# An attention and two-MoE kernel: scores before transposes, score moves joined two and two, routing steps spread over three heads, last output scaled by ScalarE

## What is computed

```python
# attention: q, k, v are (2, 8, 1152, 64); queries are averaged in pairs -> 576
q_pool = q.reshape(B, H, S // 2, 2, D).mean(axis=3)
scores = np.matmul(q_pool, k.transpose(0, 1, 3, 2)) / np.sqrt(D)
attn = softmax(scores)                       # over the 1152 keys
x = (attn @ v) -> (1152 tokens, 512)
# first MoE: the best of 8 experts for each token, at most 288 tokens each
expert_idx = np.argmax(x @ w_gate, axis=1); gate_w = softmax value of it
out[i] = gate_w[i] * (relu(x[i] @ w1[e]) @ w2[e])
# second MoE: all 8 experts for all tokens, weights balanced in 8 rounds
out += P[:, e:e + 1] * (relu(x @ w1[e]) @ w2[e])
```

## Time and profile before

| | |
|---|---|
| median of 3 runs | 1281.7 us (1281.13 to 1282.16) |
| the profiled execution's own time | 1281.55 us |
| its span | 1279.8 us |
| busy: TensorE matmul / weight load | 1247.5 us (97%) / 1167.1 us (91%) |
| busy: VectorE, ScalarE, GpSimd | 713.7 us (56%), 550.2 us (43%), 644.3 us (50%) |
| attention | 0 to about 277 us of the span |
| last head's routing, scatter and reload | about 273 to 292 us |
| the two MoE stages | from about 292 us to the end |
| granted TensorE clock, mean | 0.993 |

### The profile page before, as it was taken

The page is one execution under the profiler, slowest core; times in us unless marked ns, Lnnn a source line. Parts: engine busy times, 40 slices in busy tenths (PEclk is TensorE's granted clock), DMA queues, the critical chain, the costliest instruction groups (busy, mean ns, idle before and its releaser), DMA issues.

```text
span 1279.8 us, 23007 instructions
## 1 busy us (share of the span) xinstructions
PE 1247.5 (97%) x8056; PEld 1167.1 (91%) x8056; DVE 713.7 (56%) x1759; ACT 550.2 (43%) x1220; POOL 644.3 (50%) x529
## 2 busy tenths in 40 slices
PE   7999999968999999999999999999999999999998
PEld 6999999968999999988989989988998998998996
DVE  8999999972222222687654534534544543543552
ACT  6787777765665543323223322312412421422320
POOL 6655557519888764545335334344443532533512
PEclk9999999998999999999999999999999999999999
DMA  4364433237665652011101101001011010110101
GB/s 123 114 191 143 143 100 127 85 98 253 167 172 190 185 171 67 34 34 66 34 33 67 33 33 66 33 33 66 33 53 45 33 66 33 33 66 33 33 0 68
DMA packets 72452, 107.26 MB, mean 84 GB/s; under 512 B 7206, under 2 KB 38758, under 8 KB 72384
## 3 DMA queue, kind: packets, MB, share of 16 engines
q1 hardware_dynamic: 67792, 97.29, 23.3%
q10 hardware_dynamic: 2816, 4.72, 2.1%
q0 software_dynamic: 1776, 4.37, 0.9%
HBM read 94.92 MB, written 11.81 MB: 83 GB/s over the span
## 4 chain that ended last, share of the span: by engine, by line
PE 93%; DVE 3%; ACT 2%; issue 1%; DMA 1%; POOLq 0%; DVEq 0%; ACTq 0%
PE psum L1664 30%; PE psum L1711 26%; PE psum L1594 8%; PE psum L1577 7%; PE psum L1428 6%; PE psum L1438 6%; PE psum L1453 5%; PE psum L1653 2%; PE psum L1471 1%; ACT wsplit L696 1%; PE psum L1566 1%; DVE raw L980 1%; DVE acts L989 1%; ACT acts L696 0%; DVE small L980 0%
## 5 line engine op out<-in xcount | busy, mean ns | idle before, releaser
L1664 PE MATMUL psum<-wsplit,acts 128*128 128x512 f32 x1728 | 396.6, 390 | 0.0
L1664 PEld LDWEIGHTS psum<-wsplit,acts 128*128 128x128 f32 x1728 | 323.0, 188 | 66.1
L1711 PE MATMUL psum<-acts,wsplit 128*128 128x288 f32 x1800 | 260.9, 295 | 0.0
L1711 PEld LDWEIGHTS psum<-acts,wsplit 128*128 128x128 f32 x1800 | 247.2, 188 | 1.1
L653 POOL TENSOR_TENSOR wsplit<-raw,wsplit 128x512 fp32r<-128x512 f32 x64 | 85.9, 1365 | 297.8 <-ACT wsplit L696 297.8
L1392 DVE SCALAR_TENSOR_TENSOR x<-psum,eqr,x 128x512 f32<-128x512 f32 x126 | 94.6, 751 | 234.2 <-PE psum L1664 234.2
L643 POOL TENSOR_TENSOR wsplit<-raw,wsplit 128x512 fp32r<-128x512 f32 x109 | 140.1, 1323 | 139.6 <-ACT wsplit L696 139.6
L934 ACT ACTIVATE acts<-psum 128x288 fp32r<-128x288 f32 x240 | 92.2, 410 | 193.3 <-DVE psum L1358 118.3
L696 ACT ACTIVATE acts<-psum 128x384 fp32r<-128x384 f32 (+2 forms) x304 | 120.1, 448 | 115.8 <-PE psum L1594 56.0
L696 ACT ACTIVATE wsplit<-raw 128x512 fp32r<-128x512 f32 x301 | 169.6, 623 | 0.1
L941 ACT ACTIVATE raw<-psum 128x288 f32<-128x288 f32 x60 | 24.4, 407 | 299.8 <-PE psum L1711 299.8
(11 more groups left out here) (168 smaller groups left out, 1476.0 us busy)
## 6 DMA issues: line engine op xcount, KB each, us to landing
raw<-in_moe_w_dram SPq DMA_DIRECT2D x32, 1024.0 KB, 5.4
raw<-in_moe_w_dram SPq DMA_DIRECT2D x64, 512.0 KB, 4.2
raw<-in_k_dram SPq DMA_DIRECT2D x15, 576.0 KB, 3.7
raw<-in_q_dram SPq DMA_DIRECT2D x15, 576.0 KB, 3.9
raw<-in_v_dram SPq DMA_DIRECT2D x16, 288.0 KB, 4.5
slots_in<-zero SPq DMA_DIRECT2D x3, 1536.0 KB, 8.7
x<-slots_in ACTq DMA_DIRECT2D x7, 576.0 KB, 7.0
out_dram<-zero SPq DMA_DIRECT2D x3, 768.0 KB, 6.5
```

The costliest lines, as they stand in the source:

```text
L1664: last = mm(psum[:, bank, :], hs[a][:, l, tile * P:(tile + 1) * P], w2f[z][:, l, :], start=(l == 0 and (a, z) == (0, 0)), stop=(l == LF - ...
L1711: last = mm(psum[:, bank, 0:QN], w1f[a][:, x, cc, i * P:(i + 1) * P], src(z, cc), start=(not adds and cc == 0 and (a, z) == (0, 0)), stop= ...
```

## The change

The PSUM banks are laid out anew: `RING` becomes (0, 1, 2, 3), so that two chunks of a tile lie in neighbouring banks; the transposes take banks 4 to 6, the values bank 7. move_scores takes two chunks in one instruction and the third in another: for t below 4 chunks 0 and 1 together, then 2; for t = 4 chunk 0, then 1 and 2 together. TensorE issues scores(t + 2) before turn_probs(t); ScalarE issues exps(t + 1) before p_hi(t); VectorE issues both moves of tile t + 2 before the three p_lo(t). The transposes of the last tile take 64 rows and a 64 x 64 identity. In the routing of group 0, `one_hot` goes from head 9 t = 2 to head 10 t = 0, `slot_limit` from head 9 t = 4 to head 10 t = 1, `scatter_index` from head 10 t = 4 to head 11 t = 0. In the last head's routing `gate_input` goes ahead of `mark_expert`, `scale_output` goes from VectorE to ScalarE (one activation for each tile, after scale_logits), and `prefix(1)` goes behind the last value product. No DMA is added or removed.

```diff
...
         rs, rsr, cs, csr, gm = keep[:, 0:NT], drop[:, 0:NT], held, base[:, 0:E], pos[:, 0:4]
         g11 = den[0:1, 0:1]
         psum = ctx.enter_context(nc.psum_tensor("psum", [P, 8, 512], F32))
-        BPT, TBANKS, BPV = 3, 3, 6
-        RING = (0, 1, 2, 7)
+        BPT, TBANKS, BPV = 4, 3, 7
+        RING = (0, 1, 2, 3)
+        MOVES = ((0, 2), (2, 1))
+        MOVES_LAST = ((0, 1), (1, 2))
...
+                    if not (last and t == QT - 1):
+                        exps(*ahead(g, v, t, 1))
                     for c in range(NC):
                         p_hi(g, v, t, c)
                         if c == 0 and t == QT - 1:
                             if first:
                                 act.wait_ge(consts, 21)
                             row_sums(g)
-                    if not (last and t == QT - 1):
-                        exps(*ahead(g, v, t, 1))
...
+            def scale_output(group, bank):
+                act.wait_ge(den_done, G)
+                act.wait_ge(lgh_done, G + group - 1)
+                for n in range(*GROUPS[group]):
+                    t = n - QT
+                    last = nc.scalar.activation(x[:, t, (G - 1) * DH:G * DH], psum[:, bank, t * FD:t * FD + DH],
+                                                ACT.Copy, scale=den[:, t:t + 1])
+                last.then_inc(x_done, 1)
...
             exps(0, 0, 0)
             over_heads(head)
             evac_ot(G - 1, 0)
+            scale_output(1, BTURN)
             exp_gate(1)
             evac_ot(G - 1, 1)
             scale_rows(1)
+            scale_output(2, BTURN2)
             exp_gate(2)
             scale_rows(2)
...
-            def move_scores(g, v, t, c):
+            def move_scores(g, v, t, i):
                 b = buf(v, t)
+                c, n = (MOVES if t < QT - 1 else MOVES_LAST)[i]
+                bank = s_bank(t, c)
+                assert s_bank(t, c + n - 1) == bank + n - 1
                 if c == 0 and not (is_first(g) and t < NP):
                     dve.wait_ge(pt_ready, SCH * g + NC * (t - NP + 1))
                 if c:
                     dve.wait_ge(s_moved, SCH * g + NC * t + c)
-                dve.wait_ge(s_ready, SCH * g + NC * t + c + 1)
-                nc.vector.tensor_scalar(prob[b][:, c * CH:(c + 1) * CH], psum[:, s_bank(t, c), 0:CH],
-                                        QSCALE, low[:, b, c - 1:c] if c else None, ALU.mult, ALU.min,
-                                        accum_out=low[:, b, c:c + 1]).then_inc(s_moved, 1)
+                dve.wait_ge(s_ready, SCH * g + NC * t + c + n)
+                nc.vector.tensor_scalar(prob[b][:, c * CH:(c + n) * CH].rearrange("p (a k) -> p a k", a=n),
+                                        psum[:, bank:bank + n, 0:CH],
+                                        QSCALE, low[:, b, 0:1] if c else None, ALU.mult, ALU.min,
+                                        accum_out=low[:, b, NC - 1:NC] if c else low[:, b, 0:1]).then_inc(s_moved, n)
 
...
             def head(g, v):
                 first, last = is_first(g), is_last(g)
                 for t in range(QT):
+                    for i in (0, 1):
+                        if not (last and t >= QT - 2):
+                            move_scores(*ahead(g, v, t, 2), i)
+                    if g == CHOOSE0 and t == 1:
+                        mark_expert(0)
+                        gate_input(0)
+                    if g == PLACE0 and t == 0:
+                        one_hot(0)
+                    if g == PLACE0 and t == 1:
+                        slot_limit(0)
                     for c in range(NC):
                         p_lo(g, v, t, c)
-                        if not (last and t >= QT - 2):
-                            move_scores(*ahead(g, v, t, 2), c)
                         if t == 0 and c == 1 and not first:
                             row_sums(g - 1)
                     if t == TURN and not first:
                         scale_logits(g - 1)
                         scale_output(g - 1)
-                    if g == CHOOSE0:
-                        if t == 0:
-                            add_heads(lg[:, tiles(0), :], 0, NH)
-                            best_expert(0)
-                        elif t == 1:
-                            mark_expert(0)
-                            gate_input(0)
-                        elif t == 2:
-                            one_hot(0)
-                        elif t == 4:
-                            slot_limit(0)
+                    if g == CHOOSE0 and t == 0:
+                        add_heads(lg[:, tiles(0), :], 0, NH)
+                        best_expert(0)
                     if g == PLACE0 and t == TURN:
                         slot_number(0)
-                    if g == PLACE0 and t == QT - 1:
+                    if g == PLACE0 + 1 and t == 0:
                         scatter_index(0)
                     if g == PLACE0 and t == 1:
                         gate_weight(0)
...
-            for c in range(NC):
-                move_scores(0, 0, 0, c)
+            for i in (0, 1):
+                move_scores(0, 0, 0, i)
             q0_lo(1, slice(QA, Q))
-            for c in range(NC):
-                move_scores(0, 0, 1, c)
+            for i in (0, 1):
+                move_scores(0, 0, 1, i)
...
                 best_expert(b)
+                gate_input(b)
                 mark_expert(b)
                 one_hot(b)
-                gate_input(b)
-                scale_output(G - 1, t0, t1, bank)
                 gate_weight(b)
...
                 pe.wait_ge(exp_done, QT * g + t + 1)
                 if not (is_first(g) and m < TBANKS):
                     pe.wait_ge(pl_done, SCH * g + NC * t + c - TBANKS + 1)
+                w = qw(t)
                 for j in range(JC):
-                    last = nc.tensor.transpose(psum[:, BPT + m % TBANKS, j * P:(j + 1) * P],
-                                               prob[buf(v, t)][:, (c * JC + j) * P:(c * JC + j + 1) * P], ident[:, :])
+                    last = nc.tensor.transpose(psum[:, BPT + m % TBANKS, j * P:j * P + w],
+                                               prob[buf(v, t)][0:w, (c * JC + j) * P:(c * JC + j + 1) * P],
+                                               ident[0:w, 0:w])
                 last.then_inc(pt_ready, 1)
...
                 for t in range(QT):
                     nxt = not (last and t >= QT - 2)
                     for c in range(NC):
-                        turn_probs(g, v, t, c)
-                    for c in range(NC):
                         if nxt:
                             scores(*ahead(g, v, t, 2), c)
+                    for c in range(NC):
+                        turn_probs(g, v, t, c)
                     misc(g, v, t)
                     beside(g, v, t)
...
             LV = G - 1
             values(G - 1, LV, 1, 0, 6)
             turn_out(G - 1, 0, 2)
-            values(G - 1, LV, 1, 6, 13)
+            values(G - 1, LV, 1, 6, VSTEPS)
             prefix(1)
-            values(G - 1, LV, 1, 13, VSTEPS)
             turn_out(G - 1, 2, QT, BTURN2)
```

More of the change, by code:

```diff
@@ L1009, in scale_logits, with scale_output @@
                                         ALU.mult).then_inc(lgh_done, 1)
-            def scale_output(g, t0=0, t1=QT, bank=BTURN):
-                nc.vector.tensor_tensor(x[:, t0:t1, g * DH:(g + 1) * DH], turned(0, DH, t0, t1, bank),
-                                        den[:, t0:t1].unsqueeze(2).broadcast_to([P, t1 - t0, DH]),
+            def scale_output(g):
+                nc.vector.tensor_tensor(x[:, :, g * DH:(g + 1) * DH], turned(0, DH, 0, QT, BTURN),
+                                        den[:, :].unsqueeze(2).broadcast_to([P, QT, DH]),
                                         ALU.mult).then_inc(x_done, 1)
```

## The result

The changed kernel takes **1275.2 us** (median of 6 runs, 1273.6 to 1276.3) against 1281.6 (6 runs, 1281.0 to 1282.2) of the kernel before beside it: a ratio of 0.9949, 95% interval 0.9937 to 0.9961. It is 6.4 us faster; 12.0 were predicted. The profiled execution took 1273.6 us with a span of 1271.8, at granted clock 0.993.

The account below looks back on a forecast made before the run. TensorE's queue was taken to bound the attention, VectorE close behind. Gains of 6.5 + 2.8 + 0 + 0 + 1.4 + 1.3 = 12.0 us gave 1269.7 us from 1281.7; own range 1265.5 to 1274, with rivals A and B to 1278.

Parts of the forecast that it names:

- rival A: Last tile's transposes: narrow ones save nothing, as their weights are as wide as before; 1276.2 us, chance 0.15.
- B: Heads: VectorE becomes the bound if a tile takes 3.2 us, its head 16.0; 1276.7 us, chance 0.12.
- What bounds the kernel: Attention heads: TensorE's queue sets the time, VectorE close behind; a head goes from 16.25 to 15.6 us.
- Narrow transposes: Last tile of each head: nine transposes at half width save 0.43 us a head, 6.5 us over 15 heads.
- exps before p_hi: Tile 3 of each head: TensorE no longer waits for ScalarE's exp; 0.2 us for 14 heads, 2.8 us.
- Scores first: TensorE's order in the heads: same matmuls, nothing removed; 0, with 1 us either way in the first head.
- Joined moves: VectorE's moves of scores: at most 1.07 us up to the third chunk's move, tile 3.0; worth 0 on the path.
- Spread routing: Routing of group 0, over three heads instead of two: 1.4 us gained of 2.6, bounds 0 and 2.6.
- The end: Behind the last head: value products run through and scale_output leaves VectorE; 1.3 us gained, bounds 0.5 and 1.6.
- the sign: Sign of being right: first scatter of group 2 at 1.1 us less behind the last head's last transposes.
- The level of the clock in the first expert matmuls: First twelve expert matmuls, at the 1.2 GHz level: costed at 0 change, plus or minus 1.6 us.
- C: Heads: slower, with VectorE's tile at 3.35 us and a head of 16.6; 1285.7 us, chance 0.05.

Follow-up runs that it names:

- e1: The changed kernel with the last tile's transposes 128 rows and 128 wide again, all else as changed: 1275.6 us, ratio 0.9955 to the kernel before.
- e5: The changed kernel with ScalarE's exps behind the copies to p_hi again, TensorE's changed order kept: 1279.5 us, ratio 0.9987 to the kernel before.
- e6: The changed kernel with TensorE's transposes of a tile ahead of the scores of tile t + 2 again: 1376.0 us, ratio 1.0739 to the kernel before.
- e7: The changed kernel with three moves of one chunk each in place of the two, still ahead of p_lo: 1278.9 us, ratio 0.9979 to the kernel before.
- e10: The changed kernel with the routing steps of query group 0 back at their places in the kernel before: 1278.1 us, ratio 0.9971 to the kernel before.
- e8: The changed kernel with the last head's end as before (prefix(1), scale_output and gate_input at their old places): 1277.0 us, ratio 0.9965 to the kernel before.
- e13: The changed kernel with the last tile's transposes at 68 rows and columns and the first head's tile 0 moved by single moves: 1270.4 us, ratio 0.9916.

## Why the prediction was right or wrong

- **The total**: 6.4 us gained of 12.0 forecast. 1275.2 us lies beyond the forecast's own range, which ended at 1274, and within the whole one only because rivals A and B had been taken into it. That the time came out there is luck in part: rival A's sum is 1 us off, for a reason that the runs refute.
- **What bounds the kernel**: right. TensorE's list is the bound in steady heads before and after, and VectorE held it up in the heads with routing. But the steady period became 15.99, not 15.6.
- **Narrow transposes, 0.43 us a head, 6.5 in all**: this is the step that failed. The operations shrank nearly as predicted (109 to 62 ns), but the argument took the row for 96 rows as near enough to 64, and between them lies what costs 0.27 us at the block's ends. Measured: 0.09 a head, 1.3 us in all, so 5.2 of the 5.6 us that the sum was too good by. At 68 the term would have been nearly right: 16.08 - 15.70 = 0.38 a head. Rival A named the place and nearly the result (1276.2 us) with another reason: a floor from loading 128 weight columns. That reason is refuted: the 68-wide transposes load the same 128 columns and start 62 ns apart, the 128-wide 109. By "TensorE: Matmul & The Clock Gate" of the Trainium skill, section "LDWEIGHTS (loading the stationary operand)", the load of 128 columns is an estimate of 107 ns; as a floor under back-to-back transposes the trace doesn't agree with it.
- **exps before p_hi, 0.2 a head**: right (0.20 by e1, 0.26 by e5).
- **Scores first, 0 and 1 us either way in the first head**: right in the sum, wrong in the detail: the first transposes came late as forecast (13.47 us), 1.8 us later than before (11.64), but head 1's turn_out was no later. That VectorE's moves first need it, and that without it a head takes over 22 us instead of 16 (e6), wasn't seen.
- **Joined moves**: the durations were right (1.00 against 1.07, tile 2.94 against 3.0); worth 0 was right for steady heads. In the three with routing they are worth 2.3 us against three moves in a row (e7), together with the spreading and not on top of it.
- **Spread routing, 1.4 of 2.6**: the three heads run 1.4 us over the steady period now, so 1.2 was gained by that measure, of 1.4. By e10 it is 1.95, since bunched steps would also have taken what TensorE saves there. slot_limit, at its new place, takes 0.17 us instead of 1.07; at its old place it ended at 177.02 us, when a GpSimd subtraction (L564) had ended at 176.99, and at its new one none runs beside it, as the prediction had it:

```profile
177.32 0.17 DVE L1106 TENSOR_SCALAR st<-st 128x5 f32<-128x5 f32 x1
```

- **The end, 1.3 us**: too small, and its upper bound of 1.6 too; 1.8 by e8's median, 1.7 and 1.9 by the two pairs of profiles. The first scatter of group 2 comes 10.53 us behind the start of the last transposes (265.54 to 276.07), before 12.20 (271.23 to 283.43): 1.7 less, where 1.1 was the sign. The level of the clock in the first expert matmuls didn't change, as taken.
- Rivals B and C: VectorE's tile was under 3.2 us, so neither occurred in the changed kernel. e7, with 3.20, still ran most steady heads at TensorE's 15.98. B has 16.0 for such a tile, which is too near to TensorE's own pace to tell them apart.

The account by its terms: 1.3 (width), 2.8 (0.2 for 14 heads), 1.2 (routing), 1.8 (end, by e8) make 7.1 against the 6.4 measured. The rest is smaller than what the openings differ by, and so is the gap between the 0.4 us that e1 and the changed kernel are apart by their medians and the 1.3 that the periods make.

## What to carry to other kernels

Before a matmul or transpose is cut to 64 rows between full ones, look for a row of just that shape; here 68 rows did in 0.53 us what 64 did in 0.71, and with the first tile's single moves that kernel (e13, 1270.4 us) is 4.8 us faster than the change itself. Ask of each resource in each kind of stage who is the bound: work taken from VectorE was worth nothing in the steady heads and 2 us in three others. And when one engine's queue is reordered, ask which other queue must be reordered with it: VectorE's moves first without TensorE's scores first cost 101 us.

## What the runs showed that I had not expected

- A block of 64-row, 64-wide transposes between 128-row work pays 0.27 us at its ends (0.09 ahead, 0.05 at its first transpose, 0.12 behind); at 68, 96 and 128 nothing of the kind is seen.
- Transposes of 128 weight columns start 109, 82, 62 and 62 ns apart at 128, 96, 68 and 64 moving columns (medians of the trace's starts).
- VectorE's move with accumulator over two banks of 384 takes 0.96 us against 0.56 for one: 0.40 for the second 384 columns.
- One reordering of TensorE's queue cost 7.4% of the whole time (e6, against the kernel before), though it takes nothing away and adds nothing.
- The granted clock of a stretch doesn't tell the level at the start: the row from 10 to 20 us reads 1.00 in the changed kernel, where scores start 0.32 us apart up to 12.2 us and 0.17 from 12.9 on. The trace's record of the clock begins at 12.8 us there, and the row counts the time before it as full speed.
